# VectorE's order over the first three chunks, and one projection of TensorE put in front of a pair of transposes

## The chip, the cores and the metric

The kernel runs on one core of a Trainium2 chip. The metric is the device time of one execution in microseconds (us); lower is better. Times inside an execution come from the hardware profiler and are counted from the start of its span.

## The reference

Three stages in a row, all in float32: windowed attention, a gated MLP (here A) with RMS norm, and a second MLP (B). 2304 tokens, 512 channels.

```python
scores = scale * q @ k.T, masked to 0 <= i - j < 64
attn = exp(scores - max) / (sum + 1e-9);  x = attn @ v          # 4 batches, 8 heads, 576 x 64
xn = x / sqrt(mean(x * x) + 1e-6) * rms_g                       # MLP A: 512 -> 1536 -> 512
x = (silu(xn @ w_gate) * (xn @ w_val)) @ w_out
h = x @ w_in;  out = (h * sigmoid(1.702 * h)) @ w_out2          # MLP B: 512 -> 2048 -> 512
```

## The kernel before

**Precision.** Each float32 matrix operand is split in a high half (a cast to fp32r) and a low half (the operand minus its high half). A product is three matmuls (lines 647 to 649): high by high, low by high, high by low.

**Stages.** Tokens go through MLP A in five tiles t; tile 0 has 256 tokens and the others 512. A tile works through 12 chunks c of 128 hidden columns. A chunk has three weight blocks of 256 KB each: m = 0 gate, m = 1 value, m = 2 projection. In tile 0 each block is loaded into a buffer `raw(c % 2, m)` (line 405), cast to its high half by ScalarE (line 920) or GpSimd (line 546), and its low half is taken by VectorE (line 1215, `weights_lo_A`, counted by the semaphore `w_split`). Later tiles find all weights in place. Attention runs in steps s of 256 tokens and two heads; steps 0 to 3 stand before tile 0, steps 4 to 11 run inside tile 0 in pairs: scores of the pair (line 600) at the end of chunk 1, 3, 5, 7, transposes of its probabilities (line 614) two chunks later, and the product with v (line 628) right behind. MLP B follows tile 4.

**A chunk of tile 0 across the engines.** TensorE computes gate and value (24 matmuls of 256 columns). VectorE multiplies the gate by the inverse RMS (`scale_gate`, line 1246); ScalarE takes a tanh of that (`tanh_A`, line 996); VectorE makes the silu (`silu_A`, line 1251) and the product with the value (`hidden_A`, line 1260); ScalarE casts it (`hid_hi_A`, line 1006), VectorE subtracts (`hid_lo_A`, line 1266), and two chunks later TensorE adds it into the accumulators (`project_A`, 12 matmuls). `hidden_A(n)` waits until `hid_lo_A` of the chunk before has read the one buffer `hid`.

**An attention pair.** VectorE adds the mask and takes the row maximum (`row_max`, lines 1130 and on, one call for each step), ScalarE takes the exponentials (`exponentials`, line 881), VectorE the reciprocal of their sum and the product (`reciprocal_of_sum`, `normalise`, lines 1140 to 1147), TensorE transposes (line 614), ScalarE copies the transposed block from PSUM (`copy_probT`, line 908), TensorE multiplies by v (line 628, `probs_by_v`), which waits for that copy.

**Order.** Every engine runs one list, written out by hand in nested loops over t and c; nothing overtakes on an engine, and semaphores tie the lists together. The loops that the change and the prediction touch are these.

- TensorE, lines 747 to 768: for each chunk gate(c), val(c), the transposes of the pair, project_A(c - 2), probs_by_v of the pair, scores of the next pair. Chunk 3 of tile 0 therefore reads: gate(3), val(3), transposes of steps 4 and 5, project_A(0, 1), probs_by_v(4), probs_by_v(5), scores(6), scores(7).
- ScalarE, lines 1015 to 1041: for each chunk `exponentials` of the first step, `tanh_A`, `exponentials` of the second, `copy_probT` of both steps, `hid_hi_A(c)`, then `weights_hi_by_act(c + 3, 0)` and `(c + 3, 1)`. For chunk 3 that is tanh_A(0, 3), copy_probT(4), copy_probT(5), hid_hi_A(0, 3), casts of chunk 6.
- GpSimd, lines 565 to 582: casts block 2 of chunk c + 3 in chunk c's turn.
- SyncE, lines 434 to 462: issues all loads of weights, q, k and v in one queue. In chunk c's turn it loads the three blocks of chunk c + 3, and then q and k of the pair after next. It waits before each load (lines 402 to 405):

```python
def load_wA(c, m):
    if c >= 2:
        sp.wait_ge(w_split, splitsA(c - 2, m))
```

`splitsA(c, m)` gives the place of block (c, m) in VectorE's order of low halves, since `w_split` only counts. Block (4, 2) has the buffer of block (2, 2), so its load waits for `weights_lo_A(2, 2)`, and every load behind it in the queue waits too.

Of the kernel before, what the change touches and what calls it, by code (L numbers as in the profile page):

```python
# [23 lines left out]
def fused_attention_mlps(nc, q_t, k_t, v_win, w_a, rms_g, w_b, out):  # L24
# [8 lines left out]
    LAG = 2  # L33
# [33 lines left out]
    with ExitStack() as ctx:  # L67
# [208 lines left out]
        FIRST_SPLITS = ((0, 0), (0, 1), (1, 0), (1, 1), (2, 0), (0, 2), (2, 1), (1, 2), (2, 2))  # L276

        def splitsA(c, m):
            return FIRST_SPLITS.index((c, m)) + 1 if c < 3 else 3 * c + m + 1

# [303 lines left out]
        def _(pe):  # L584
# [162 lines left out]
            for t in range(NA):  # L747
                for c in range(CA + LAG if t < NA - 1 else CA):
                    scored = pair_with_scores_at(t, c)
                    transposed = pair_with_scores_at(t, c - 2)  # L750
                    if c < CA and (t > 0 or c > 0):
                        gate(t, c)
                        if t == 0 and c == 1:
                            sum_squares(0)
                        val(t, c)
                    if transposed is not None:
                        transpose_probs(transposed)
                        transpose_probs(transposed + 1)
                    if c >= LAG:
                        project_A(t, c - LAG)  # L760
                    if transposed is not None:
                        probs_by_v(transposed, CA * t + c)
                        probs_by_v(transposed + 1)
                    if scored is not None:
                        scores(scored)
                        scores(scored + 1)
                    if c == SUMSQ_AT and t + 1 < NA:
                        sum_squares(t + 1)
# [99 lines left out]
        def _(act):  # L868
# [146 lines left out]
            for t in range(NA):  # L1015
                for c in range(CA):
# [22 lines left out]
                    if t == 0 and c + 3 < CA:  # L1039
# [75 lines left out]
        def _(dve):  # L1115
# [167 lines left out]

            for t in range(NA):
                for c in range(CA):
# [5 lines left out]
                    if t == 0 and c != 1:  # L1291
                        scale_gate(c)
                    if t == 0 and c == 0:
                        scale_gate(1)
                        weights_lo_A(2, 1)
# [3 lines left out]
                    if split is not None and c > 0 and c != 2:  # L1299
# [13 lines left out]
                    if split is not None and c == 2:  # L1313
                        weights_lo_A(split, 0)
                    if split is not None and c > 0:
                        weights_lo_A(split, 1)
                    if t == 0 and c == 0:
                        weights_lo_A(1, 2)
# [142 lines left out]
```

## Time and profile before

| | |
|---|---|
| Median of 3 runs | 904.4 us (903.55 to 904.43) |
| The profiled execution: its own time | 903.96 us |
| The profiled execution: span of the core | 901.3 us |
| TensorE busy | 889.2 us, 99% of the span |
| VectorE busy | 539.1 us, 60% |
| ScalarE busy | 400.2 us, 44% |
| GpSimd busy | 81.0 us, 9% |
| Mean granted clock of TensorE, as a share of full | 0.998 |

The 2.66 us between span and time lie around the profiled span. A row of the timeline gives start, duration, engine, source line, operation, output <- input, its size, how many were merged, and in brackets how long the engine was idle before it and what ended that. Durations of neighbours overlap a little, so a step on an engine is read from start to start. TensorE's matmuls are pipelined, and their step from start to start is what counts.

### The profile page before, as it was taken

What the parts mean: (1) busy time and instruction counts of PE and PEld (TensorE: products, weight loads), DVE (VectorE), ACT (ScalarE), POOL (GpSimd) and SP (SyncE); (2) the same over time, 40 slices, a digit from 0 to 9 for tenths busy, and PEclk for the clock granted to TensorE, in tenths of its full rate; (3) what the DMA queues carried; (4) which work ended last, traced back from release to release, by engine and by line L of the source; (5) the groups of instructions that cost most, each with busy time, mean ns of one, the idle gap of its engine ahead of it and who ended that gap; (6) DMA issues with size and microseconds to landing.
All of it is one profiled execution on the core that took longest, in us unless ns stands there. A gap on an engine that the chain in (4) does not pass through costs nothing.

```text
span 901.3 us, 14698 instructions
## 1 busy us (share of the span) xinstructions
PE 889.2 (99%) x5368; PEld 771.5 (86%) x5368; DVE 539.1 (60%) x1256; ACT 400.2 (44%) x944; POOL 81.0 (9%) x111
## 2 busy tenths in 40 slices
PE   8899999999999999999999999999999999999998
PEld 7799888888888888888888899999999999999997
DVE  6896633334333343333336578887788788867663
ACT  6666333343333433334123354545464554545442
POOL 5234001030010300112000000000000000000000
PEclk9999999999999999999999999999999999999999
DMA  7673111102111021100500222121432121241201
GB/s 243 217 218 94 51 51 51 50 24 74 51 50 52 24 74 50 51 25 1 186 1 24 94 95 70 63 78 47 164 117 94 48 77 65 69 143 48 70 24 70
DMA packets 41078, 69.75 MB, mean 77 GB/s; under 512 B 3632, under 2 KB 13872, under 8 KB 41008
## 3 DMA queue, kind: packets, MB, share of 16 engines
q1 hardware_dynamic: 39600, 67.12, 22.9%
q10 hardware_dynamic: 1408, 1.70, 0.5%
q8 instruction: 43, 0.70, 0.3%
q14 instruction: 27, 0.22, 0.1%
HBM read 59.38 MB, written 9.44 MB: 76 GB/s over the span
## 4 chain that ended last, share of the span: by engine, by line
PE 93%; DVE 3%; ACT 2%; issue 1%; POOL 0%; ACTq 0%; POOLq 0%
PE ps L647 16%; PE ps L648 15%; PE ps L649 15%; PE ps L839 7%; PE ps L840 7%; PE ps L838 7%; PE ps L781 7%; PE ps L777 7%; PE ps L779 6%; PE ps L628 2%; PE ps L600 2%; PE ps L614 1%; DVE w_all L1215 1%; ACT prob L881 1%; DVE sig L1251 0%
## 5 line engine op out<-in xcount | busy, mean ns | idle before, releaser
L647 PE MATMUL ps<-x_hi,w_all 128*128 128x512 f32 (+1 forms) x480 | 179.3, 373 | 0.0
L649 PE MATMUL ps<-x_lo,w_all 128*128 128x512 f32 (+1 forms) x480 | 176.7, 368 | 0.0
L648 PE MATMUL ps<-x_hi,w_all 128*128 128x512 f32 (+1 forms) x480 | 176.7, 368 | 0.0
L840 PE MATMUL ps<-w2out,hB 128*128 128x512 f32 x288 | 113.0, 392 | 0.0
L839 PE MATMUL ps<-w2out,hB 128*128 128x512 f32 x288 | 112.9, 392 | 0.0
L838 PE MATMUL ps<-w2out,hB 128*128 128x512 f32 x288 | 112.0, 389 | 0.0
L647 PEld LDWEIGHTS ps<-x_hi,w_all 128*128 128x128 f32 x480 | 90.4, 188 | 18.1 <-issue 3.0
L649 PEld LDWEIGHTS ps<-x_lo,w_all 128*128 128x128 f32 x480 | 90.4, 188 | 15.3
L648 PEld LDWEIGHTS ps<-x_hi,w_all 128*128 128x128 f32 x480 | 90.4, 188 | 14.4
L1251 DVE SCALAR_TENSOR_TENSOR sig<-sig,ps 128x512 f32<-128x512 f32 x48 | 32.9, 686 | 107.1 <-ACT sig L996 107.1
L647 PE MATMUL ps<-h_hi,w_all 128*128 128x512 f32 (+1 forms) x240 | 90.4, 377 | 1.9 <-DVE hid L1260 1.7
L648 PE MATMUL ps<-h_hi,w_all 128*128 128x512 f32 (+1 forms) x240 | 88.9, 370 | 0.0
L649 PE MATMUL ps<-h_lo,w_all 128*128 128x512 f32 (+1 forms) x240 | 88.9, 370 | 0.0
L1260 DVE TENSOR_TENSOR hid<-ps,sig 128x512 f32<-128x512 f32 (+1 forms) x59 | 37.9, 642 | 66.3 <-PE ps L649 52.7
L781 PE MATMUL ps<-xcB_even,w2in 128*128 128x384 f32 x224 | 75.2, 336 | 0.0
L777 PE MATMUL ps<-xcB_even,w2in 128*128 128x384 f32 x224 | 75.2, 336 | 0.0
L1006 ACT CAST h_hi<-hid 128x512 fp32r<-128x512 f32 (+1 forms) x60 | 34.8, 580 | 90.8 <-DVE hid L1260 90.8
L779 PE MATMUL ps<-xcB_even,w2in 128*128 128x384 f32 x224 | 75.1, 335 | 0.0
L996 ACT ACTIVATE sig<-ps 128x512 f32<-128x512 f32 x48 | 28.6, 597 | 103.6 <-PE ps L649 103.4
L840 PEld LDWEIGHTS ps<-w2out,hB 128*128 128x128 f32 x288 | 54.0, 188 | 11.4
L839 PEld LDWEIGHTS ps<-w2out,hB 128*128 128x128 f32 x288 | 54.0, 188 | 10.4
L838 PEld LDWEIGHTS ps<-w2out,hB 128*128 128x128 f32 x288 | 54.1, 188 | 10.2
(148 smaller groups left out, 1556.0 us busy)
## 6 DMA issues: line engine op xcount, KB each, us to landing
wstage<-in_w_b SPq DMA_DIRECT2D x48, 512.0 KB, 3.5
wstage<-in_w_a SPq DMA_DIRECT2D x36, 256.0 KB, 3.3
vwin<-in_v_win SPq DMA_DIRECT2D x32, 256.0 KB, 3.7
kwin<-in_k_t SPq DMA_DIRECT2D x32, 160.0 KB, 3.3
x2raw<-x_scratch SPq DMA_DIRECT2D x3, 1536.0 KB, 6.7
out_dram<-yB SPq DMA_DIRECT2D x18, 256.0 KB, 4.5
qtok<-in_q_t SPq DMA_DIRECT2D x34, 128.0 KB, 2.6
x_scratch<-wstage SPq DMA_DIRECT2D x3, 1024.0 KB, 4.2
```

What stands on the lines that cost most here:

```text
L647: pe.matmul(out_, w[:, 0, cols], xh, start=first, stop=False, **flags)
L648: pe.matmul(out_, w[:, 1, cols], xh, start=False, stop=False, **flags)
L649: return pe.matmul(out_, w[:, 0, cols], xl, start=False, stop=last, **flags)
L777: pe.matmul(out_, w2in[:, g % 2, 0, a_, cols], x[:, b_, 0, d, :], start=fresh and d == 0, stop=False, skip_group_check=True)
L779: pe.matmul(out_, w2in[:, g % 2, 1, a_, cols], x[:, b_, 0, d, :], start=False, stop=False, skip_group_check=True)
L781: ins = pe.matmul(out_, w2in[:, g % 2, 0, a_, cols], x[:, b_, 1, d, :], start=False, stop=last, skip_group_check=True)
L838: pe.matmul(y, h[:, rows], w[:, 0, chunk, :], start=(p == 0 and first), stop=False)
L839: pe.matmul(y, h[:, rows], w[:, 1, chunk, :], start=False, stop=False)
L840: ins = pe.matmul(y, hB_of(g, chunk, 1)[:, rows], w[:, 0, chunk, :], start=False, stop=last)
L1006: nc.scalar.copy(h_hi[:, c % RING, 0:TILES_A[t][1]], hid[:, 0:TILES_A[t][1]]).then_inc(hidA_hi, 1)
L1251: nc.vector.scalar_tensor_tensor(out=silu_of(t, c), in0=silu_of(t, c), scalar=1.0, in1=scaled_of(c) if t == 0 else gate_of(t, c), op0=ALU. ...
L1260: nc.vector.tensor_tensor(hid[:, 0:w], val_of(t, c), silu_of(t, c), ALU.mult).then_inc(hidA_made, 1)
```

## The change

Four edits, with the constant list that belongs to them.

1. TensorE: in chunk 3 of tile 0, project_A(0, 1) comes in front of the transposes of steps 4 and 5.
2. VectorE: chunks 0 to 2 of tile 0 leave the loop and are written out. The low halves of blocks (2, 2), (3, 0), (3, 1) and (3, 2) come later than they did, silu and hidden of chunk 1 come ahead of them, row_max(5) comes behind hid_lo_A(0, 1) and scale_gate(2), and the normalisation of both steps comes ahead of silu_A(0, 2). The low halves of chunk 4 stand at the end, ahead of scale_gate(3). Chunks 3 and on are as before.
3. ScalarE: the casts of blocks (4, 0) and (4, 1) move from behind hid_hi_A(0, 1) to behind hid_hi_A(0, 2), where those of (5, 0) and (5, 1) follow them.
4. `FIRST_SPLITS` lists VectorE's new order of low halves, so the counts that the loads and the matmuls wait for change with it: the load of block (4, 2) still waits for the low half of (2, 2), which now is the eleventh instead of the ninth.

```diff
--- before.py
+++ after.py
@@ -273,10 +273,11 @@
         def raw(u, m):
             return wstage[:, (3 * u + m) * DM:(3 * u + m + 1) * DM]
 
-        FIRST_SPLITS = ((0, 0), (0, 1), (1, 0), (1, 1), (2, 0), (0, 2), (2, 1), (1, 2), (2, 2))
+        FIRST_SPLITS = ((0, 0), (0, 1), (1, 0), (1, 1), (2, 0), (0, 2), (2, 1), (1, 2), (3, 0), (3, 1),
+                        (2, 2), (3, 2), (4, 0), (4, 1), (4, 2))
 
         def splitsA(c, m):
-            return FIRST_SPLITS.index((c, m)) + 1 if c < 3 else 3 * c + m + 1
+            return FIRST_SPLITS.index((c, m)) + 1 if c < 5 else 3 * c + m + 1
 
         CASTS_BY_ACT = ((0, 1), (1, 1), (2, 0), (2, 1)) + tuple((c, m) for c in range(3, CA) for m in range(2))
         CASTS_BY_POOL = ((0, 0), (1, 0), (0, 2), (1, 2)) + tuple((c, 2) for c in range(2, CA))
@@ -753,10 +754,12 @@
                         if t == 0 and c == 1:
                             sum_squares(0)
                         val(t, c)
+                    if (t, c) == (0, 3):
+                        project_A(t, c - LAG)
                     if transposed is not None:
                         transpose_probs(transposed)
                         transpose_probs(transposed + 1)
-                    if c >= LAG:
+                    if c >= LAG and (t, c) != (0, 3):
                         project_A(t, c - LAG)
                     if transposed is not None:
                         probs_by_v(transposed, CA * t + c)
@@ -1036,7 +1039,10 @@
                     hid_hi_A(t, c)
                     if c == SUMSQ_AT and t + 1 < NA:
                         inverse_rms(t + 1)
-                    if t == 0 and c + 3 < CA:
+                    if t == 0 and c == 2:
+                        weights_hi_by_act(4, 0)
+                        weights_hi_by_act(4, 1)
+                    if t == 0 and c != 1 and c + 3 < CA:
                         weights_hi_by_act(c + 3, 0)
                         weights_hi_by_act(c + 3, 1)
                     if t == NA - 1 and 4 <= c < 4 + COMBOS:
@@ -1281,22 +1287,46 @@
                         nc.vector.tensor_scalar(x2stage(t)[:, j, 0:n], acc_of(t, j), 0.5, None,
                                                 ALU.mult).then_inc(accA_evacuated[1], 1)
 
+            scale_gate(0)
+            scale_gate(1)
+            weights_lo_A(2, 1)
+            silu_A(0, 0)
+            hidden_A(0, 0)
+            silu_A(0, 1)
+            weights_lo_A(1, 2)
+            hid_lo_A(0, 0)
+            hidden_A(0, 1)
+            weights_lo_A(3, 0)
+            weights_lo_A(3, 1)
+            row_max(EARLY)
+            hid_lo_A(0, 1)
+            scale_gate(2)
+            row_max(EARLY + 1)
+            reciprocal_of_sum(EARLY)
+            normalise(EARLY)
+            reciprocal_of_sum(EARLY + 1)
+            normalise(EARLY + 1)
+            silu_A(0, 2)
+            hidden_A(0, 2)
+            weights_lo_A(2, 2)
+            weights_lo_A(3, 2)
+            hid_lo_A(0, 2)
+            for m in range(3):
+                weights_lo_A(4, m)
+
             for t in range(NA):
-                for c in range(CA):
+                for c in range(3 if t == 0 else 0, CA):
                     scored = pair_with_scores_at(t, c - 1)
                     if scored is not None:
                         row_max(scored)
                         row_max(scored + 1)
                     split = c + 2 if t == 0 and c + 2 < CA else None
-                    if t == 0 and c != 1:
+                    if t == 0:
                         scale_gate(c)
-                    if t == 0 and c == 0:
-                        scale_gate(1)
-                        weights_lo_A(2, 1)
                     if scored is not None:
                         reciprocal_of_sum(scored)
                         normalise(scored)
-                    if split is not None and c > 0 and c != 2:
+                    if split is not None:
                         weights_lo_A(split, 0)
                     silu_A(t, c)
                     hidden_A(t, c)
@@ -1310,12 +1340,8 @@
                     if scored is not None:
                         reciprocal_of_sum(scored + 1)
                         normalise(scored + 1)
-                    if split is not None and c == 2:
-                        weights_lo_A(split, 0)
-                    if split is not None and c > 0:
+                    if split is not None:
                         weights_lo_A(split, 1)
-                    if t == 0 and c == 0:
-                        weights_lo_A(1, 2)
                     hid_lo_A(t, c)
                     if split is not None:
                         weights_lo_A(split, 2)
```

## Rows read from the trace of the kernel before

**Rows 1.** The page, part 4: shares by engine of the chain that ended last.

```profile
PE 93%; DVE 3%; ACT 2%; issue 1%; POOL 0%; ACTq 0%; POOLq 0%
```

**Rows 2.** Timeline of TensorE (PE), 26 to 43 us: start, duration, line, idle before.

```profile
26.95 0.28 PE L648 MATMUL ps<-x_hi,w_all 128*128 128x256 f32 x1
27.07 0.28 PE L649 MATMUL ps<-x_lo,w_all 128*128 128x256 f32 x1
29.02 0.35 PE L647 MATMUL ps<-h_hi,w_all 128*128 128x256 f32 x1 [1.67 <-DVE hid L1260]
...
34.55 0.65 PE L614 MATMUL ps<-ident,prob 128*128 128x128 f32 x4 [0.99 <-DVE prob L1147]
36.77 1.04 PE L614 MATMUL ps<-ident,prob 128*128 128x128 f32 x4 [1.57 <-DVE prob L1147]
...
38.04 0.41 PE L649 MATMUL ps<-h_lo,w_all 128*128 128x256 f32 x1
38.25 0.41 PE L647 MATMUL ps<-h_hi,w_all 128*128 128x256 f32 x1
...
40.30 1.15 PE L628 MATMUL ps<-probT,vwin 128*64 128x64 f32 x32
...
42.42 0.39 PE L647 MATMUL ps<-x_hi,w_all 128*128 128x256 f32 x1
```

**Rows 3.** Table by windows: busy time (x instructions) of PE, PEld, DVE, ACT, POOL; PEclk; DMA.

```profile
37.00:39.50 2.50, 2.50 (x13) 2.50 (x12) 2.50 (x6) 0.46 (x2) 0.00 (x0) 0.50 0.39 112
40.25:40.50 0.25, 0.25 (x7) 0.20 (x8) 0.25 (x2) 0.25 (x1) 0.00 (x0) 0.88 0.60 156
42.40:91.00 48.60, 47.06 (x502) 45.55 (x498) 38.99 (x119) 32.40 (x96) 20.49 (x28) 1.00 0.53 157
```

**Rows 4.** Timeline of VectorE (DVE), 24 to 43 us.

```profile
24.61 0.43 DVE L1251 SCALAR_TENSOR_TENSOR sig<-sig 128x256 f32<-128x256 f32 x1 [0.30 <-ACT sig L996]
...
25.41 0.68 DVE L1215 TENSOR_TENSOR w_all<-wstage,w_all 128x512 fp32r<-128x512 f32 x1
26.01 0.83 DVE L1266 TENSOR_TENSOR h_lo<-hid,h_hi 128x256 fp32r<-128x256 f32 x1
26.77 1.31 DVE L1215 TENSOR_TENSOR w_all<-wstage,w_all 128x512 fp32r<-128x512 f32 x2
...
30.74 0.28 DVE L1130 CUSTOM_DVE_ANT_0 prob<-ps,mask 128x128 f32<-128x128 f32 x1
...
32.43 0.41 DVE L1246 TENSOR_TENSOR sig<-ps,hid 128x256 f32<-128x256 f32 x1
33.38 0.17 DVE L1140 TENSOR_SCALAR rrec<-rsum 128x4 f32<-128x4 f32 x1 [0.54 <-ACT prob L881]
...
33.80 0.69 DVE L1147 TENSOR_TENSOR prob<-prob,rrec 128x512 f32<-128x512 f32 x1
34.41 0.83 DVE L1251 SCALAR_TENSOR_TENSOR sig<-sig 128x256 f32<-128x256 f32 x1
...
36.02 0.69 DVE L1147 TENSOR_TENSOR prob<-prob,rrec 128x512 f32<-128x512 f32 x1
```

**Rows 5.** Timeline of ScalarE (ACT), 24 to 43 us.

```profile
26.73 1.26 ACT L920 CAST w_all<-wstage 128x512 fp32r<-128x512 f32 x2 [0.79 <-DMA wstage<-in_w_a]
...
29.46 0.62 ACT L920 CAST w_all<-wstage 128x512 fp32r<-128x512 f32 x1 [0.15 <-DMA wstage<-in_w_a]
30.37 0.62 ACT L920 CAST w_all<-wstage 128x512 fp32r<-128x512 f32 x1 [0.28 <-DMA wstage<-in_w_a]
31.70 0.40 ACT L881 ACTIVATE prob<-prob,nmax 128x128 f32<-128x128 f32 x1 [0.71 <-DVE nmax L1130]
...
39.55 1.06 ACT L908 COPY probT<-ps 128x512 f32<-128x512 f32 x2
```

**Rows 6.** Timeline of GpSimd (POOL), 24 to 43 us.

```profile
28.80 1.15 POOL L546 CAST w_all<-wstage 128x512 fp32r<-128x512 f32 x1 [2.23 <-DMA wstage<-in_w_a]
```

**Rows 7.** Timeline of the queue of SyncE (SP), 26 to 27 us.

```profile
26.12 1.28 SPq L405 DMA_DIRECT2D wstage<-in_w_a  x3
```

## The prediction, made before the changed kernel was run

> **What bounds the kernel now.** I read the page first, then TensorE's timeline, then the lists of the other engines around its gaps. TensorE holds 93% of the chain that ended last [rows 1], so time is won or lost only where TensorE stands still or runs slowly. From 42.42 us, where gate(4) starts, it does neither: up to 91 us it is busy 47.06 of 48.60 us at the full clock [rows 3]. A shift of gate(4) should therefore reach the end one for one, and the question is when gate(4) starts.
>
> Between 27.35 and 42.42 us the reader should see three gaps and a slow stretch [rows 2]. TensorE waits 1.67 us for hidden_A(0, 1) before project_A(0, 0), 0.99 us for the normalisation of step 4, and 1.57 us for that of step 5. Then its matmuls step by 0.21 us (38.04 to 38.25) where they stepped by 0.12 (26.95 to 27.07). The granted clock is 0.50 from 37.0 to 39.5 us, which is 1.2 GHz, and is on its way back to 2.4 GHz at 40.25 to 40.50 [rows 3]. So it fell near 36.9 us, after TensorE had stood still for most of 3 us, and came back about 3.4 us after the restart at 36.77. Those 3.4 us at half speed cost 1.7 us. All of it lies ahead of probs_by_v(4) at 40.30.
>
> **Where the list of VectorE helps.** Steps are read from start to start: 0.60 us for a low half of 512 columns, 0.34 for an operation of 256 columns (a row's 0.42 less the overlap of 0.08), 0.80 for silu and hidden together (24.61 to 25.41), 0.85 for one row_max (half of 30.74 to 32.43), 0.42 for the reciprocal pair and 0.61 for normalise (33.38, 33.80, 34.41) [rows 4]. Nothing changes until hidden_A(0, 0) is out at 25.41. Then silu(0, 1) takes until 25.75, weights_lo(1, 2) until 26.35, hid_lo(0, 0) until 27.1 if I keep its stretched step of 0.76 (26.01 to 26.77; GpSimd casts beside it), and hidden(0, 1) ends at 27.55. TensorE can start project_A(0, 0) at 27.7: 1.3 us earlier than 29.02. Then project_A(0, 0), gate(3), val(3) and, by the move on TensorE, project_A(0, 1) are 48 matmuls at 0.12, until 33.45, at the full clock. The move covers the 0.99 us gap with 1.44 us of work.
>
> VectorE goes on from 27.5: low halves (3, 0) and (3, 1), whose casts are done at 27.99 [rows 5], until 28.7; row_max(4) 29.55; hid_lo(0, 1) 29.9; scale_gate(2) 30.25; row_max(5) 31.1. ScalarE starts exponentials 0.1 us behind a row_max and needs 1.68 us for a step (31.70 in [rows 5] to the reciprocal at 33.38 in [rows 4]): 29.65 to 31.35, then tanh(0, 2) 0.3, then step 5 until 33.35. Its reciprocal and normalise end at 34.4. TensorE transposes step 4 at 33.45 to 33.9, stands still 0.5 us, and transposes step 5 at 34.45 to 34.9. That is 2.3 us ahead of before (36.77).
>
> **Where the gain stops.** The next work on TensorE is now probs_by_v(4), which waits for copy_probT(4). Three lists meet in front of that copy.
>
> - VectorE: silu(0, 2) and hidden(0, 2) stand behind normalise(5), until 35.2, and weights_lo(2, 2) behind them, until 35.85. Before, this low half was the first of the pair at 26.77, done near 27.45 [rows 4]. It is 8.4 us later.
> - SyncE: the load of block (4, 2) waits for that low half. Queued behind it are the loads of (5, 0), (5, 1), (5, 2), q and k of steps 6 and 7, and chunk 6. All of them shift from 27.5 and later to 35.85 and later.
> - ScalarE: behind hid_hi(0, 2) stand four casts, the last two of blocks (5, 0) and (5, 1), and behind those tanh(0, 3) and copy_probT(4).
>
> For the loads I take the same pattern from before: three loads in a row from 26.12 [rows 7], released by a low half that ended at 26.09. The first block's cast started at 28.80 [rows 6], the second's at 29.46 and the third's at 30.37, both released by the DMA [rows 5]. That is 2.7, 3.4 and 4.3 us after the low half. So (4, 2) can be cast at 38.55, (5, 0) at 39.25, (5, 1) at 40.15. ScalarE's cast of (5, 1) ends at 40.75. The other branch ends with it: GpSimd casts (4, 2) until 39.2 or, at 1.15 us, 39.7; weights_lo(4, 2) and scale_gate(3), which now stands behind it, take 1.0 to 1.1 more, until 40.3 to 40.8. Then tanh(0, 3) 0.35, and probs_by_v 0.75 us behind the start of the copies (39.55 in [rows 5], 40.30 in [rows 2]): **41.85 us against 40.30, so 1.55 us later**. Error from both sides: without the slowing by GpSimd 0.4 earlier; with a slower transfer behind the cast 0.5 later.
>
> TensorE meanwhile has nothing from 34.9 to 41.85, seven us. A gap pattern half as long brought it to half clock before, so I take it that it restarts at 1.2 GHz. Before, probs_by_v, the scores and gate(4) ran at full clock. Now two pairs of groups that take 2.1 us at full clock (40.30 to 42.42) and the first matmuls of chunk 4 run slowly for 3.4 us as before: 1.7 us lost. Bounds: 0.9 us if the clock is back after some 1.8 us, 2.6 if it takes 5.2. Before lost the same 1.7 us, but inside the stretch that ends at 40.30, so it is already in that number. The Trainium skill, page "TensorE: Matmul & The Clock Gate", section "Terms", prices the throttle as throttled time times one half. Counted with the standstill, from some 37 to 45.3 us, its rule gives an estimated 4.2 us where before had 1.7, so 2.5 us net of before and a total near 4.0. The row above charges only the stretch in which matmuls run, and the sum goes by that.
>
> **The other edits.** The casts of (4, 0) and (4, 1) on ScalarE are 1.2 us in a place where ScalarE then waits for the load of (5, 0) until 39.25: nothing. If that load were early, they would be in front of the copy with 1.2 us. Low halves of chunk 3 are ready for gate(3) and val(3) by 28.7 and 29.1 us is when TensorE wants the first: nothing. q and k of step 6 are issued near 37.5 and wanted near 44: nothing. Casts of chunk 6 come behind loads issued near 39.4, and evacuate_o(4), which val(4) waits for, stands behind them on ScalarE near 45, with val(4) near 47: nothing, with 2 us to spare. After that every wait hangs on TensorE's own scores, so I see nothing that gives time back.
>
> **Sum.** 1.55 + 1.7 = 3.25 us. gate(4) starts near 45.7 instead of 42.42. Against the profiled execution 903.96 + 3.25 = 907.2; the median shown is 0.44 above that execution, so the forecast is **907.6 us**. From this kernel's spread, 0.2% (1.8 us) is about what can be told from no change.
>
> **The rivals.**
>
> A, the forecast: load queue and cold restart, 2.4 to 4.3 us, 906.8 to 908.7. Chance 0.70.
>
> B: the delay of probs_by_v is there, but the clock stays up or is back at once. Then +1.5 us, 905.9, inside 0.2%. For it: TensorE stood still 1.67 us at 27.35 without losing the clock. Against: the gap is now four times that. Chance 0.09.
>
> C: the loads hold nothing, because blocks (4, 2) to (5, 1) are in place early. VectorE's list alone then gives 35.2 + 0.6 + 0.6 + 0.34 + 1.8 + 0.42, scale_gate(3) at 39.0, tanh, copy, probs_by_v at 40.1. With the cold restart that is +1.5, without it -0.2: the same. Against it: the wait in load_wA reads exactly the low half that is moved. Chance 0.06.
>
> D: the queue stays behind. If loads of chunk 6 take 2 us more than by the pattern (q and k share the engines), ScalarE holds evacuate_o(4) and the exponentials of step 6, and 1 to 2 us come on top: 909 to 910. Chance 0.11.
>
> E, faster: probs_by_v(4) starts before 38.5 and no cold stretch remains. The price is what the gaps cost before, up to 1.67 + 0.99 + 1.57 + 1.7 = 5.9 us; a start at 38 gives about 902. It decides only if tanh(0, 3) does not wait for a load and VectorE has scale_gate(3) out by 37.3. Its own list from hidden(0, 2) at 35.2 holds 3.8 us. Chance 0.04.
>
> **Numbers.** Slower by over 0.2%: A and D, 0.81. Within 0.2%: B and C, 0.15. Faster: 0.04. The range leaves out E, C and the far half of D: 905.6 to 909.3.
>
> **What would show it.** Right: project_A(0, 0) near 27.7, line 614 at 33.5 and 34.5, all steps of 0.12 before that; SyncE's load of (4, 2) near 35.9; ScalarE's casts of (5, 0) and (5, 1) released by the DMA; line 628 near 41.9 behind the copy; a granted clock of 0.50 from about 37 to 45; gate(4) near 45.7. Wrong: an early load of (4, 2), a copy of step 4 before 39.5, a clock of 1.00 at 43 us, or TensorE gaps beyond 46 us that before did not have or had and lost.

## The result

The changed kernel takes 907.75 us (median of 6 runs, 906.85 to 908.04) against 904.17 us (median of 6, 903.55 to 904.43): ratio 1.0040, 95% interval 1.0030 to 1.0051. That is slower by 0.4%, 3.6 us, where 3.25 us on top of 904.4 were forecast. The profiled span is 905.1 us against 901.3, 3.8 us more. One execution of pe_only below, the profiled one, took 1103.57 us with a mean granted clock of 0.752; its ratio leaves this one out, and pe_only_b is one more execution of the same kernel, profiled.

The line numbers of the changed kernel are a little higher: 648 to 650 are the three matmuls, 601 the scores, 615 the transposes, 629 the product with v, 1221 the low halves, 1252 scale_gate, 1266 hidden_A, 1272 hid_lo_A, 923 and 547 the casts by ScalarE and GpSimd, 911 the copies, 999 tanh, 406 the loads.

TensorE's timeline after, the lines that answer to [rows 2]:

```profile
27.89 0.35 PE L648 MATMUL ps<-h_hi,w_all 128*128 128x256 f32 x1 [0.54 <-DVE hid L1266]
...
33.70 0.60 PE L615 MATMUL ps<-ident,prob 128*128 128x128 f32 x4
34.57 0.66 PE L615 MATMUL ps<-ident,prob 128*128 128x128 f32 x4 [0.27 <-DVE prob L1153]
42.42 1.97 PE L629 MATMUL ps<-probT,vwin 128*64 128x64 f32 x32 [7.19 <-ACT probT L911]
44.32 1.99 PE L601 MATMUL ps<-kwin,qtok 64*64 64x128 f32 x32
46.24 0.58 PE L648 MATMUL ps<-x_hi,w_all 128*128 128x256 f32 x1
...
48.12 0.28 PE L648 MATMUL ps<-x_hi,w_all 128*128 128x256 f32 x1
...
56.56 1.17 PE L629 MATMUL ps<-probT,vwin 128*64 128x64 f32 x32 [0.22 <-ACT probT L911]
```

The last two of these lines are the start of val(4) and the product of step 6. Before, they are:

```profile
43.95 0.28 PE L647 MATMUL ps<-x_hi,w_all 128*128 128x256 f32 x1
...
52.73 1.17 PE L628 MATMUL ps<-probT,vwin 128*64 128x64 f32 x32 [0.55 <-ACT probT L908]
```

The first gap is down from 1.67 to 0.54 us, the second is gone, the third is 0.27 us: step 5 is transposed 2.2 us earlier than before. Then comes a gap that before did not have, 7.19 us in front of line 629, released by ScalarE's copy. The product and the scores, 2.12 us before (40.30 to 42.42), take 3.82 us (42.42 to 46.24). gate(4) starts at 46.24 instead of 42.42: 3.82 us later. The first matmul of tile 1 starts at 95.09 against 91.27, again 3.82 us. Between the two points two small things cancel. The first matmuls of gate(4) are slow as well, until 47 us, so val(4) is 4.17 us late (48.12 against 43.95). And TensorE waits 0.4 us for the copies of the later pairs where before it waited 0.8, so the product of step 6 is 3.83 us late.

The windows, as in [rows 3] (PEclk stands ahead of the DMA share), show the slow stretch:

```profile
36.50:36.75 0.25, 0.00 (x0) 0.00 (x0) 0.25 (x2) 0.25 (x1) 0.00 (x0) 1.00 0.00 0
37.00:42.40 5.40, 0.00 (x0) 0.01 (x1) 3.24 (x6) 2.15 (x5) 1.23 (x2) 0.50 0.91 299
42.42:46.24 3.82, 3.82 (x65) 3.37 (x65) 1.98 (x5) 2.40 (x6) 0.31 (x1) 0.50 1.03 351
46.24:47.00 0.76, 0.76 (x7) 0.76 (x4) 0.63 (x5) 0.13 (x1) 0.56 (x2) 0.50 0.71 257
47.00:92.00 45.00, 44.04 (x477) 42.71 (x476) 36.56 (x113) 29.67 (x90) 17.05 (x26) 1.00 0.53 159
```

The clock is at its full 2.4 GHz at 36.5 us and at 1.2 GHz from 37 to 47 us, which is 10 us. TensorE had work for 4.6 of them (42.42 to 47).

The queue of loads, the low halves on VectorE, the casts on GpSimd and ScalarE, and the copies, as in [rows 4 to 7]:

```profile
25.75 1.10 DVE L1221 TENSOR_TENSOR w_all<-wstage,w_all 128x512 fp32r<-128x512 f32 x1
...
35.23 1.28 DVE L1221 TENSOR_TENSOR w_all<-wstage,w_all 128x512 fp32r<-128x512 f32 x2
...
39.29 0.69 DVE L1221 TENSOR_TENSOR w_all<-wstage,w_all 128x512 fp32r<-128x512 f32 x1 [1.24 <-POOL w_all L547]
39.90 0.42 DVE L1252 TENSOR_TENSOR sig<-ps,hid 128x256 f32<-128x256 f32 x1
```

```profile
35.94 1.28 SPq L406 DMA_DIRECT2D wstage<-in_w_a  x3
```

```profile
38.64 0.61 POOL L547 CAST w_all<-wstage 128x512 fp32r<-128x512 f32 x1 [8.41 <-DMA wstage<-in_w_a]
```

```profile
35.66 1.13 ACT L923 CAST w_all<-wstage 128x512 fp32r<-128x512 f32 x2
39.27 0.62 ACT L923 CAST w_all<-wstage 128x512 fp32r<-128x512 f32 x1 [2.48 <-DMA wstage<-in_w_a]
40.87 0.62 ACT L923 CAST w_all<-wstage 128x512 fp32r<-128x512 f32 x1 [0.98 <-DMA wstage<-in_w_a]
41.39 0.41 ACT L999 ACTIVATE sig<-sig 128x256 f32<-128x256 f32 x1
41.71 1.05 ACT L911 COPY probT<-ps 128x512 f32<-128x512 f32 x2
```

This is the chain in order of time. The low half (2, 2) is the first of the pair at 35.23 on VectorE. SyncE, held by it, issues three loads from 35.94. GpSimd casts (4, 2) at 38.64, after 8.41 us of waiting for that load. ScalarE, done with chunk 4's casts, waits 2.48 us for block (5, 0) and 0.98 us more for (5, 1), both released by the DMA. Only behind these stand tanh(0, 3) at 41.39 and the copies at 41.71. VectorE's branch ended earlier: scale_gate(3) started at 39.90, so it was not the one that came last.

### The profile page after: what moved, and what is told of

Same layout as the page of the kernel before. It is cut to its first block, busy times and chain, and to the rows that moved or that the text cites. A ratio compares the mean times of both kernels' runs of the same rounds, so it can differ in the third digit from the quotient of the medians.

```text
span 905.1 us, 14698 instructions
## 1 busy us (share of the span) xinstructions
PE 889.6 (98%) x5368; PEld 772.2 (85%) x5368; DVE 539.4 (60%) x1256; ACT 400.2 (44%) x944; POOL 79.2 (9%) x111
## 4 chain that ended last, share of the span: by engine, by line
PE 93%; DVE 3%; ACT 2%; issue 1%; DMA 0%; POOL 0%; SPq 0%; ACTq 0%; DVEq 0%; POOLq 0%
PE ps L648 15%; PE ps L650 15%; PE ps L649 15%; PE ps L842 7%; PE ps L843 7%; PE ps L841 7%; PE ps L784 6%; PE ps L780 6%; PE ps L782 6%; PE ps L629 2%; PE ps L601 2%; PE ps L615 1%; ACT prob L884 1%; DVE w_all L1221 1%; DMA wstage<-in_w_a 0%
## 5 line engine op out<-in xcount | busy, mean ns | idle before, releaser
L843 PEld LDWEIGHTS ps<-w2out,hB 128*128 128x128 f32 x288 | 54.0, 188 | 11.3
L884 ACT ACTIVATE prob<-prob,nmax 128x128 f32<-128x128 f32 x136 | 52.8, 391 | 23.1 <-DVE nmax L1136 23.1
L842 PEld LDWEIGHTS ps<-w2out,hB 128*128 128x128 f32 x288 | 54.1, 188 | 10.4
```

What stands on the lines that cost most here:

```text
L842: pe.matmul(y, h[:, rows], w[:, 1, chunk, :], start=False, stop=False)
L843: ins = pe.matmul(y, hB_of(g, chunk, 1)[:, rows], w[:, 0, chunk, :], start=False, stop=last)
L884: ins = nc.scalar.activation(prob_block(s, h, m), prob_block(s, h, m), ACT.Exp, bias=nmax[:, s % EARLY, n:n + 1], scale=-1.0, accum_out=rs ...
```

## Experiments

All kernels were timed in turn with the kernel before; a ratio is to its runs on the same chip, with a 95% interval. copies_first, copies_proj, early_warm and pe_only_b ran on a second chip. Where the intervals of two kernels overlap, the ratios alone do not tell them apart. "Product" is the start of the first product with v in tile 0, "tile 1" the start of its first matmul of 512 columns, both from the one profiled execution, for pe_only that of pe_only_b.

| kernel | ratio (interval) | product, us | tile 1, us |
|---|---|---|---|
| before | | 40.30 | 91.27 |
| the change | 1.0040 (1.0030 to 1.0051) | 42.42 | 95.09 |
| lists_only | 1.0040 (1.0027 to 1.0052) | 42.42 | 94.92 |
| pe_only; pe_only_b | 1.0010 (1.0001 to 1.0019) | 40.19 | 92.42 |
| early_22 | 1.0025 (1.0014 to 1.0035) | 40.15 | 93.03 |
| warm | 1.0032 (1.0021 to 1.0044) | 42.48 | 94.19 |
| early_warm | 1.0018 (1.0010 to 1.0027) | 40.10 | 91.92 |
| copies_first | 1.0006 (0.9998 to 1.0015) | 35.92 | 91.44 |
| copies_proj | 1.0014 (1.0005 to 1.0023) | 35.94 | 93.85 |
| copies_all | 1.0009 (1.0000 to 1.0019) | 36.32 | 92.00 |
| pool_lo | 1.0035 (1.0022 to 1.0047) | 37.90 | 95.32 |
| pool_only | 1.0042 (1.0028 to 1.0056) | 42.22 | 95.87 |
| copies_before | 0.9987 (0.9978 to 0.9995) | 38.78 | 90.30 |

**The two halves of the change: lists_only and pe_only.** lists_only is the changed kernel with TensorE's order of before:

```diff
-                    if (t, c) == (0, 3):
-                        project_A(t, c - LAG)
                     if transposed is not None:
                         transpose_probs(transposed)
                         transpose_probs(transposed + 1)
-                    if c >= LAG and (t, c) != (0, 3):
+                    if c >= LAG:
                         project_A(t, c - LAG)
```

> The changed kernel with TensorE's order put back: transposes of steps 4 and 5 ahead of project_A(0, 1). My theory (the loss is made by VectorE's late low half (2, 2), the queue of loads behind it and the casts in front of copy_probT(4)): the same late copy near 41.7 and line 628 near 42.4, so the same time as the changed kernel, 3.8 us over before, within 0.5 us. Rival (TensorE's move makes a good part of the loss): at least 1 us faster than the changed kernel.

It has the ratio of the whole change and the product at the same 42.42 us. The loss is made by the lists of VectorE and ScalarE, and on top of them TensorE's move adds nothing. pe_only is the other half alone, the same diff the other way round on the kernel before.

> The kernel before with only TensorE's move: project_A(0, 1) ahead of the transposes of steps 4 and 5; VectorE's, ScalarE's and the load order stay. My theory (the pair's product waits for ScalarE's copies, wherever TensorE's own work stands): the gap of 0.99 us goes, but step 5 is still normalised at 36.7, and copy_probT(4) still comes at 39.55 behind tanh(0, 3), so line 628 stays at 40.3. The projection no longer stands in the stretch from 37.5 to 40.2, so TensorE is idle there and the product, the scores and the first matmuls of chunk 4 run at 1.2 GHz: 1.0 to 1.7 us slower than before, gate(4) near 44. Rival (the move is a gain by itself, covering the gap): gate(4) about 1 us earlier than 42.42, 1 us faster.

The trace is that of pe_only_b.

> The same kernel as pe_only, for a profile with the clock at its usual levels. My theory: line 628 near 40.3, product and scores at 1.2 GHz, gate(4) near 44 and 1 us more at tile 1. Rival: gate(4) at or ahead of 42.4.

```profile
34.77 0.60 PE L614 MATMUL ps<-ident,prob 128*128 128x128 f32 x4
36.70 0.66 PE L614 MATMUL ps<-ident,prob 128*128 128x128 f32 x4 [1.33 <-DVE prob L1149]
40.19 1.98 PE L628 MATMUL ps<-probT,vwin 128*64 128x64 f32 x32 [2.83 <-ACT probT L910]
42.10 1.99 PE L600 MATMUL ps<-kwin,qtok 64*64 64x128 f32 x32
```

As my theory had it: the gap of 0.99 us is filled (the transposes start at 34.77), the product does not move, TensorE now stands still for 2.83 us in front of it, and the product and the scores run at half clock, 1.9 us each instead of 1.1. gate(4) starts at 44.02, tile 1 1.15 us later than before, and the ratio says 0.9 us (0.1 to 1.7). A move that fills one gap has opened another one behind it, in front of the same late copy.

**The load queue: early_22.** The low half (2, 2), which holds the load of block (4, 2), moves up in VectorE's list.

```diff
             weights_lo_A(3, 1)
+            weights_lo_A(2, 2)
             row_max(EARLY)
...
             hidden_A(0, 2)
-            weights_lo_A(2, 2)
             weights_lo_A(3, 2)
```

> The changed kernel with weights_lo_A(2, 2) moved up on VectorE, from behind hidden_A(0, 2) to behind weights_lo_A(3, 1), ahead of row_max(4). That releases the load of block (4, 2) near 29.5 us instead of 35.9. My theory (the load queue holds the copy): VectorE's attention work slips 0.6 us, casts of chunk 5 no longer wait for a DMA, scale_gate(3) comes near 39.0, line 628 near 40.1 instead of 42.4, still after a long standstill and so at 1.2 GHz: 2 to 2.5 us faster than the changed kernel, 1.3 to 1.8 us slower than before. Rival (the wait for the load is covered by something else, VectorE's list or ScalarE's four casts): line 628 stays near 42 or goes to 42.6 with the slip, same time as the changed kernel.

```profile
40.15 1.98 PE L629 MATMUL ps<-probT,vwin 128*64 128x64 f32 x32 [4.38 <-ACT probT L911]
```

```profile
36.20 2.17 ACT L923 CAST w_all<-wstage 128x512 fp32r<-128x512 f32 x4
39.11 0.42 ACT L999 ACTIVATE sig<-sig 128x256 f32<-128x256 f32 x1 [0.74 <-DVE sig L1252]
```

ScalarE casts the four blocks of chunks 4 and 5 in one go at 36.20, with no wait for a DMA. The copy is released by tanh(0, 3), which now waits for scale_gate(3) on VectorE. The product starts 2.27 us earlier than in the changed kernel and tile 1 2.06 us earlier; by the ratios it is 1.4 us, where 2 to 2.5 were expected. That shows the queue of loads as the last wait of the change, and VectorE's own list close behind it: at 40.15 us the product has only come back to its old place.

**The clock: warm and early_warm.** In warm, matmuls whose result nobody reads fill the standstill of the changed kernel.

```diff
                         transpose_probs(transposed + 1)
+                    if (t, c) == (0, 3):
+                        pe.wait_ge(gate_scaled, 3)
+                        keep_busy(4, 26)
```

> The changed kernel with 26 idle-filling matmuls of 128 columns on TensorE behind the transposes of steps 4 and 5, into the free PSUM bank 4 (they wait for scale_gate(2)); nothing waits for their result. They fill about 7 us of the standstill from 35.1 to 42.4. My theory (of the 3.8 us, 1.7 to 2.1 are the half clock behind the standstill): line 628 stays at 42.4, the product and the scores take 2.1 us instead of 3.8, the granted clock stays at 1.00, and the kernel is 1.7 to 2.2 us faster than the changed one, about 1.7 us slower than before. Rival (the clock costs nothing, or it falls in spite of them): same as the changed kernel, or slower where they run past 42.4.

```profile
34.95 5.97 PE L726 MATMUL ps<-ones 128*128 128x128 f32 x52
42.48 1.17 PE L629 MATMUL ps<-probT,vwin 128*64 128x64 f32 x32 [1.57 <-ACT probT L914]
43.59 1.10 PE L601 MATMUL ps<-kwin,qtok 64*64 64x128 f32 x32
...
46.62 0.36 PE L648 MATMUL ps<-x_hi,w_all 128*128 128x256 f32 x1 [0.30 <-issue]
```

```profile
44.67 1.30 ACT L926 CAST w_all<-wstage 128x512 fp32r<-128x512 f32 x2 [1.46 <-DMA wstage<-in_w_a]
45.88 0.64 ACT L880 COPY xT<-ps 128x256 f32<-128x256 f32 x2
```

The product and the scores take 2.14 us again (42.48 to 44.62, where gate(4) starts) with a granted clock of 1.00, against 3.82 at half clock. gate(4) is 1.62 us earlier than in the changed kernel. Only 0.90 us of it arrives at tile 1, and 0.7 by the ratios: my 1.7 to 2.2 us were wrong. A part of the reason stands in the second fence: ScalarE waits 1.46 us for the blocks of chunk 6, casts them, and only then copies the outputs of steps 4 and 5 (line 880). val(4) waits for that copy, and TensorE stands still for 0.30 us, until 46.62. Its waits for the copies of later pairs are 0.8 us in all, where the changed kernel has 0.4. In the changed kernel these waits were hidden behind the slow matmuls. The wait in front of val(4) is the one that I had priced at nothing, and at more as rival D. early_warm does the same with early_22 (19 instead of 26 calls):

> early_22 with 19 idle-filling matmuls of 128 columns behind the transposes of steps 4 and 5 (bank 4, no reader). My theory: line 628 stays at 40.15, the product and the scores take 2.1 us instead of 3.8, so gate(4) starts at 42.3 as before. The casts of chunk 6, released by the DMA near 42.7, then hold evacuate_o(4) and with it val(4) by 0.5 to 1 us: 0.4 to 1 us slower than before, 0.9 to 1.5 faster than early_22. Rival (the clock is the whole rest): equal to before within 0.2 us.

The product is at 40.10 and tile 1 at 91.92, 0.65 us behind before, with a wait of 0.65 us in front of val(4) and 0.7 us of later waits for copies, about as long as before. So in that profile the three terms (late product, clock, chunk 6's casts) account for the change's 3.8 us: 2.06, 1.11 and 0.65. The timed runs do not bear this out as well. The profiled execution, 903.71 us, was the fastest of 11, and their median is 905.13, 1.8 us behind before. By the ratios early_warm gains 0.6 us on early_22, with overlapping intervals, where 0.9 to 1.5 were expected. That the late load costs time does not hang on one profile: all six spans of the changed kernel are 904.7 us or more, and seven of early_22's eight are 903.9 or less. The size of the clock's share rests on profiles alone. What the other runs lose is not settled.

**Was the gain there to be had? copies_first.** In early_22 the product waits for a copy that stands behind tanh(0, 3) in ScalarE's list and needs nothing from it. From early_22, on ScalarE:

```diff
-                    if multiplied is not None:
+                    if multiplied is not None and (t, c) != (0, 4):
                         evacuate_o(multiplied)
...
+                    if (t, c) == (0, 2):
+                        copy_probT(EARLY)
+                        copy_probT(EARLY + 1)
-                    if transposed is not None:
+                    if transposed is not None and (t, c) != (0, 3):
                         copy_probT(transposed)
                         copy_probT(transposed + 1)
                     hid_hi_A(t, c)
+                    if (t, c) == (0, 3):
+                        evacuate_o(EARLY)
+                        evacuate_o(EARLY + 1)
```

and on SyncE the loads of q and k of steps 6 and 7 in chunk 0's turn.

> The kernel with weights_lo_A(2, 2) early and three more moves. ScalarE: copy_probT(4) and (5) go from behind tanh(0, 3) to ahead of hid_hi_A(0, 2), and evacuate_o(4) and (5) ahead of the casts of chunk 6. SyncE: q and k of steps 6 and 7 are loaded in chunk 0's turn, ahead of the blocks of chunk 4. My theory (the product of the pair waits for nothing but the place of the copies in ScalarE's list): line 628 near 36.0 instead of 40.15, right behind hidden_A(0, 2), no standstill over 1 us before it and the clock at 1.00; gate(4) near 38.1. From there VectorE's list is the bound: val(4) near 41, row_max(6) near 42 against 42.56 before, so most of the lead is lost in front of the transposes of steps 6 and 7; 0.5 to 2 us faster than before, 2.5 to 4 faster than early_22. Rival (TensorE is the bound from 42 on, as the page's 99% suggests): the whole lead of 4 us stays, 4 us faster than before. Second rival: TensorE now stands still in later chunks and loses the clock there, no faster than before.

```profile
35.92 1.31 PE L632 MATMUL ps<-probT,vwin 128*64 128x64 f32 x32
...
42.17 0.36 PE L651 MATMUL ps<-x_hi,w_all 128*128 128x256 f32 x1 [2.29 <-issue]
...
48.00 0.60 PE L618 MATMUL ps<-ident,prob 128*128 128x128 f32 x4
49.81 0.66 PE L618 MATMUL ps<-ident,prob 128*128 128x128 f32 x4 [1.22 <-DVE prob L1162]
...
52.70 1.17 PE L632 MATMUL ps<-probT,vwin 128*64 128x64 f32 x32 [0.81 <-ACT probT L914]
53.80 1.10 PE L604 MATMUL ps<-kwin,qtok 64*64 64x128 f32 x32
```

The product comes at 35.92 us, 4.4 us ahead of before and at full clock. Before, the scores of steps 8 and 9 started at 53.83; here they start at 53.80. The lead is lost in 18 us: 2.29 us in front of val(4), 1.22 for the normalisation of step 7, 0.81 for its copy. The gap in front of val(4) shows no releaser; ScalarE's evacuate_o(4), which it waits for, came at 41.43 behind hid_hi_A(0, 3), and that was released by VectorE's hidden_A(0, 3). What holds step 7 is VectorE. The first line is its row_max(6) before, the second that of copies_first:

```profile
42.56 0.29 DVE L1130 CUSTOM_DVE_ANT_0 prob<-ps,mask 128x128 f32<-128x128 f32 x1 [0.44 <-PE ps L600]
```

```profile
42.54 0.29 DVE L1145 CUSTOM_DVE_ANT_0 prob<-ps,mask 128x128 f32<-128x128 f32 x1
```

Before, VectorE waited 0.44 us for the scores. Here the scores are there by 38.3 us, 4 us earlier, and row_max(6) still starts at 42.54, because VectorE works through its list until then. From there on it is the same list: normalise(7) starts at 49.09 before, at 48.93 here. So of a lead of 4 us nothing came through to step 7. From 27 to 54 us VectorE is busy 24.60 us of 27 here, and 25.03 before. In this stretch it is VectorE's list, as it is written, and not TensorE that sets the pace. Whether another order on VectorE would let the pair through earlier was not tried. The rival that the 99% of the page suggests (the whole lead stays) is wrong. My own 0.5 to 2 us were wrong too: the kernel is as fast as before. The second rival had this time by another way, a lost clock, and the profile has a mean granted clock of 1.000.

copies_proj puts the projection ahead of the transposes for all four pairs:

> copies_first, and TensorE's project_A(c - 2) stands ahead of the transposes for all four pairs of tile 0 (chunks 3, 5, 7, 9) and not only the first. My theory: with VectorE as the bound, 1.44 us of projection fills part of TensorE's wait for the normalisation of each pair: at least as fast as copies_first and up to 1 us faster. Rival: the product with v then comes 1.44 us later behind the copy with nothing in front of it, and it is 0 to 2 us slower.

In the profiled execution it is slower, as the rival had it: tile 1 at 93.85 us against 91.44. In chunk 5 the transposes of step 6 start at 49.60 instead of 48.00, and the wait for the copy grows from 0.81 to 2.23 us; the scores behind it take 1.99 us, at half clock. But this execution, 906.33 us, was the second slowest of 11. The medians are 0.5 us apart (904.24 against 903.70) and the intervals overlap, so the timed runs show only that the move does not help.

**Less work for VectorE: pool_lo and pool_only.** pool_only is the kernel before, and GpSimd, which is idle most of the time, takes the low half of block 2 of chunks 3 to 11:

```diff
                 nc.gpsimd.tensor_copy(slotA(c)[:, m, 0, :], raw(c % 2, m)).then_inc(w_hi_made, 1)
+                if c >= 3:
+                    pool.wait_ge(w_hi_made, casts_so_far(False, c, m))
+                    nc.gpsimd.tensor_tensor(slotA(c)[:, m, 1, :], raw(c % 2, m), slotA(c)[:, m, 0, :].bitcast(F32),
+                                            ALU.subtract).then_inc(w_lo_by_pool, 1)
...
             def weights_lo_A(c, m):
+                if c >= 3 and m == 2:
+                    return
```

The loads and matmuls that wait for these low halves wait for the new count w_lo_by_pool.

> The kernel before with the low halves of block 2 of chunks 3 to 11 taken by GpSimd instead of VectorE, nothing else. My theory: row_max(4) comes 0.6 us earlier (the low half (3, 2) stood ahead of it), scale_gate(3) and with it the copies 1.2 to 1.8 us earlier, later pairs no longer wait for the copies (0.55 and 0.24 us before): 1 to 2.5 us faster than before. Rival (stretched operations): same as before or up to 1 us slower.

pool_lo adds this to copies_first, with two more moves on ScalarE and VectorE.

> copies_first with the low halves of block 2 of chunks 3 to 11 taken by GpSimd (right behind its cast of the same block) instead of VectorE, evacuate_o(4) and (5) on ScalarE ahead of the casts of chunk 5, and scale_gate(3) ahead of the low half (4, 1). My theory (VectorE's list is what holds the pair's chain and eats the lead in tile 0): VectorE has 0.6 us less work for each chunk, val(4) no longer waits 2.3 us, the lead of 4 us at the scores of step 6 is kept in good part: tile 1 starts 2 to 4 us earlier than the 91.27 of before, 2 to 4 us faster than before. Rival (two engines on the same memory slow each other, so VectorE's operations stretch by what it was spared): same as copies_first.

My theory was wrong in both, and the rivals named a cause that the trace shows, but far too small a price: pool_only is 4.0 us slower than before by the medians (up to 1 us foreseen), and pool_lo 2.6 us slower than copies_first by the ratios (the same foreseen). Groups of VectorE from 27 to 80 us (mean ns behind the busy time), in the kernel before:

```profile
L1251 DVE SCALAR_TENSOR_TENSOR sig<-sig 128x256 f32<-128x256 f32 x8 | 4.2, 520 | 0.0
...
L1147 DVE TENSOR_TENSOR prob<-prob,rrec 128x512 f32<-128x512 f32 x8 | 6.1, 766 | 0.3
```

and in pool_only, where the same two are lines 1262 and 1156, with GpSimd's new operation:

```profile
L1156 DVE TENSOR_TENSOR prob<-prob,rrec 128x512 f32<-128x512 f32 x8 | 7.8, 977 | 0.3
...
L1262 DVE SCALAR_TENSOR_TENSOR sig<-sig 128x256 f32<-128x256 f32 x7 | 6.0, 861 | 0.0
```

```profile
L552 POOL TENSOR_TENSOR w_all<-wstage,w_all 128x512 fp32r<-128x512 f32 x9 | 12.4, 1376 | 0.7
```

The silu takes 861 ns instead of 520 on average, the normalisation 977 instead of 766. GpSimd needs 1376 ns for what VectorE does in about 720, and while it does it, operations of VectorE with two inputs in SBUF get longer. One pair of them in pool_only:

```profile
51.43 1.29 POOL L552 TENSOR_TENSOR w_all<-wstage,w_all 128x512 fp32r<-128x512 f32 x1
```

```profile
51.65 1.61 DVE L1156 TENSOR_TENSOR prob<-prob,rrec 128x512 f32<-128x512 f32 x1
```

The normalisation takes 1.61 us instead of 0.69 and ends 0.54 us behind GpSimd's subtraction. Tile 1 comes 4.6 us later than before. Not all of it is the price of the longer operations: the granted clock is 0.50 from 38.5 to 42 us while TensorE works throughout, and in pool_lo from 39 to 41. How the 4.6 us divide was not taken apart.

**Only the copies: copies_before and copies_all.** copies_before is the kernel before with the copies of both steps ahead of tanh, for the four pairs of tile 0:

```diff
+                    if t == 0 and transposed is not None:
+                        copy_probT(transposed)
+                        copy_probT(transposed + 1)
                     if (t, c) != (0, 1):
                         tanh_A(t, c)
...
-                    if transposed is not None:
+                    if transposed is not None and t > 0:
                         copy_probT(transposed)
                         copy_probT(transposed + 1)
```

> The kernel before with copy_probT of both steps ahead of tanh for all four pairs of tile 0, nothing else. My theory: the copies fall where ScalarE waits for scale_gate, so nothing is put off; in chunk 3 nothing is won, since TensorE's cold project_A(0, 1) ends at 40.2 as well; in chunks 5 and 7 the 0.55 and 0.24 us of wait go: tile 1 starts 0.3 to 0.8 us earlier, a gain under 0.1%. Rival (VectorE is the bound and gives it back): tile 1 at 91.27 and no gain.

```profile
36.76 0.66 PE L614 MATMUL ps<-ident,prob 128*128 128x128 f32 x4 [1.59 <-DVE prob L1150]
...
38.78 1.15 PE L628 MATMUL ps<-probT,vwin 128*64 128x64 f32 x32
...
49.80 0.66 PE L614 MATMUL ps<-ident,prob 128*128 128x128 f32 x4 [0.68 <-DVE prob L1150]
...
51.81 1.15 PE L628 MATMUL ps<-probT,vwin 128*64 128x64 f32 x32
```

```profile
37.08 1.06 ACT L908 COPY probT<-ps 128x512 f32<-128x512 f32 x2
39.22 0.42 ACT L996 ACTIVATE sig<-sig 128x256 f32<-128x256 f32 x1 [1.08 <-DVE sig L1249]
```

This one is faster than both kernels, by little: 0.9987 (0.9978 to 0.9995), 1.2 us (0.5 to 2.0) less than before, where under 0.9 were expected. The copies run at 37.08, in a stretch where ScalarE waited for scale_gate(3), and tanh(0, 3) still starts at 39.22, so nothing is put off. In the profiled execution the clock stays at full, the projection ends by 38.7 and the product is 1.5 us earlier than before, where I had expected nothing from chunk 3. But this lead does not last: step 7 is transposed at 49.80, while in the kernel before all eight transposes of steps 6 and 7 start at 49.71. What is left is that step 6 is transposed by then and that the wait of 0.55 us for the copies is gone. The product of step 6 starts at 51.81 against 52.73, and 0.97 us is left at tile 1. copies_all joins all moves of ScalarE and SyncE, the early low half (2, 2) and scale_gate(3) ahead of the low half (4, 1) with the change:

> copies_first without any work for GpSimd, with evacuate_o(4) and (5) on ScalarE ahead of the casts of chunk 5, scale_gate(3) ahead of the low half (4, 1), and copy_probT ahead of tanh for the other pairs of tile 0 as well (chunks 5, 7, 9). My theory (waits for ScalarE's order are removable, VectorE's work is not): val(4) starts 2 us earlier, the products of steps 6 and 8 no longer wait for the copies (0.8 and 0.4 us in copies_first), and what is left are TensorE's waits for the normalisation: tile 1 starts 0.5 to 2 us ahead of the 91.27 of before. Rival (VectorE's list alone sets tile 0): tile 1 within 0.5 us of 91.4, same as copies_first.

Tile 1 is at 92.00 and the kernel is no faster than before, so my 0.5 to 2 us were wrong; the rival had the time nearly (within 0.5 of 91.4). val(4) does start at 39.96, 2.2 us earlier than in copies_first, and step 6 is transposed at 46.58 instead of 48.00. But row_max(6) starts at 42.75, and the transposes of step 7 wait 2.80 us for their normalisation, until 50.03: a longer lead on TensorE only lengthens its wait for VectorE at step 7.

## Why the prediction was right

**VectorE's early part.** Right, within 0.25 us: project_A(0, 0) at 27.89 (27.7 foreseen), transposes at 33.70 and 34.57 (33.45 and 34.45), the low half (2, 2) done near 35.9 (35.85). hidden_A(0, 1) was released by hid_lo(0, 0) after a stretched low half (1, 2), 1.10 us at 25.75, where I had put the stretch on the next operation.

**The load queue holds the copy.** Right, and shown by early_22. The first load was cast at 38.64 (38.55 foreseen) and the second at 39.27 (39.25). The third was the term that was too small: the pattern from before gave 40.15, and it was cast at 40.87. With its successors the product came at 42.42 instead of 41.85. So the delay was 2.12 us and not 1.55. That is 0.57 us over, just beyond the 0.5 that the prediction gave to a slower transfer, and this is the term that was mis-sized most. Why the third load was slow stays open. At 39 to 40 us, ahead of it, the core's DMA engines moved 206 GB/s, where they moved 334 and 367 in the two microseconds from 29 to 31 us before, when the third block of the pattern came.

**Half clock for the product and the scores.** Right in direction, and at gate(4) in size: the shift there is 3.82 us with 2.12 of delay in it, so 1.70 us for the clock, 1.7 foreseen. But the slow stretch did not end 3.4 us after the restart, as before and as the term had it; it lasted 4.6 us, until 47, and took in the start of gate(4). At val(4) the shift is 4.17 us, 2.05 of it for the clock. What counts is the time in which matmuls run slowly. The rule of the Trainium skill, page "TensorE: Matmul & The Clock Gate", section "Terms", would charge the 10 us of throttle with an estimated 5.0 us, less 1.7 for before, so 3.3, and the trace, with 2.05, does not agree with it. warm showed that it is not a saving to be had alone: with the clock kept up, only 0.9 us came back at tile 1.

**The edit costed at nothing.** The casts of chunk 6 in front of val(4) were costed at nothing, with 2 us to spare. That held in the changed kernel, but only because the product and the scores ran at half clock. With full clock there was no spare time: warm and early_warm waited for it.

**Nothing gives it back.** Not quite: the 0.35 us that the slow start of gate(4) cost beyond the forecast came back in shorter waits for copies, of which before had 0.8 us. So the shift is 3.82 us at 46.24, 3.82 at tile 1 and 3.8 in the span, against 3.25 in the sum. That the forecast of 907.6 lies within 0.2 us of the median is in part luck. The delay was 0.57 us too small; the two errors behind it, in the clock's length and in what comes back, cancelled; the base of 904.4 was 0.2 us above the median of six runs; and the medians lie 3.6 us apart where the profiled spans lie 3.8.

**An inexact reading of before.** The prediction says that before's half clock "cost 1.7 us" in the stretch up to 40.30, and rival E counted these 1.7 us as something to be won. Of the 76 runs of the kernel before beside the experiments, 40 had a mean granted clock of 1.000, 35 one of 0.997 or 0.998 and one of 0.947. The profiled one, with its 3.4 us at half clock in 901, has 0.998. So in about half of the runs the kernel before seems not to fall to half clock; only one of its executions has a trace, so this rests on the means. On the first chip the median span is 901.5 us for either kind (23 and 26 runs), on the second 901.1 against 901.5 (17 and 9). By these medians the cold stretch costs the kernel before 0 to 0.4 us and not 1.7. The copy explains it: pe_only_b, with no projection between the transposes and the product, still has the product at 40.19. The reading did not touch the sum, which took 40.30 as it stood.

## What to carry to other kernels

Ahead of moving work up on the bound engine, find out what the next instruction behind it waits for, and on which list that stands; a filled gap in front of a wait that does not move only moves the gap, and can cost the clock as well. When a low-priority operation is put off, ask what it frees: here 0.6 us of VectorE's work released a buffer, a queue of loads in order, two casts and the copy behind them, and putting it off by 8.4 us cost 2 us. An engine busy 60% of the span can be the bound of a stretch of 27 us, and a lead won ahead of it on TensorE is lost within that stretch. A move on an engine that truly waits (the copies on ScalarE) was small, 1.2 us, but stayed.

## What was not expected of the hardware

**GpSimd beside VectorE.** A subtraction of two SBUF inputs on GpSimd took 1.38 us against 0.72 on VectorE, and VectorE's own silu went from 520 to 861 ns on average, with 9 such operations in 53 us. The Trainium skill, page "SBUF — State Buffer", section "SBUF: two separate sides", says that a VectorE operation with two SBUF inputs and a GpSimd operation that reads SBUF block each other for a whole instruction; the trace agrees with it, in these means and in the pair at 51.43 us above, where VectorE's operation ended 0.54 us behind GpSimd's, which is most of its usual 0.69. The prediction had used only the small version of this, a stretched step of 0.76 us.

**The clock with the same gaps.** The one trace of the kernel before has a stretch at half clock from 37 to 40 us, and the mean clocks of its runs (1.000 in 40, 0.997 or 0.998 in 35) say that others seem to have none. copies_before, with the same two gaps ahead of 36.76 us to within 0.05 us, ran its transposes at full clock there (0.66 us for four) where [rows 2] has 1.04. In lists_only, where TensorE stood still from 36.7 to 42.42 us, the clock was still at 1.00 at 37 to 40 us. These traces do not tell what decides whether such gaps cost the clock.
